# A routed-expert stage in a three-stage kernel: two buffers for the split relu output, three PSUM banks for y, unused tiles signalled ahead of the last product with w2, last y stores by SyncE

## What is computed

```python
# stage A: attention, half the heads with a plain window of 32, half with a dilated one
scores = where(mask, q @ k.T / 8, -1e9); x = softmax(scores) @ v      # -> (4, 576, 512)
# stage B: a router with memory, then one expert of 8 for each token
e = argmax(logits) if s == 0 or sigmoid(x @ w_local) < 0.5 else prev_e
h = maximum(x[b, s] @ w1[e], 0.0)        # 512 -> 1024
out[b, s] = p[e] * (h @ w2[e])           # 1024 -> 512
# stage C: a gated projection
gate = sigmoid(causal_conv(x, conv_w, 5 taps)); y = (gate * (x @ w_val)) @ w_out
```

## Time and profile before

| | us |
|---|---|
| median of 3 runs | 605.35 |
| lowest, highest | 600.86, 609.49 |
| the profiled execution | 606.63 |
| its span, first to last instruction | 604.9 |
| TensorE busy | 550.4 (91%) |
| VectorE, ScalarE, GpSimd busy | 265.5, 214.9, 246.6 |
| mean granted clock of TensorE | 0.955 of full speed |

### The profile page before, as it was taken

One profiled execution on the slowest core, in us unless ns is written; L12 is line 12 of the kernel. 1 busy time (PEld: TensorE's weight loads), 2 busy tenths in 40 slices (PEclk: granted clock), 3 DMA queues, 4 the chain that ended last, 5 costly groups with the idle time before them and its releaser, 6 DMA issues.

```text
span 604.9 us, 9972 instructions
## 1 busy us (share of the span) xinstructions
PE 550.4 (91%) x3274; PEld 466.9 (77%) x3274; DVE 265.5 (44%) x833; ACT 214.9 (36%) x478; POOL 246.6 (41%) x145
## 2 busy tenths in 40 slices
PE   7899999974789997999999999999699587999997
PEld 3789899862568886788888888878587386999986
DVE  4577777745722122021212221221112579998720
ACT  3577777741012112121212121221112454665421
POOL 1000000471177466636175577575743526522210
PEclk9799999985899999799999999999999788999999
DMA  5758489868179996978588797999761522210112
GB/s 179 183 167 223 138 267 321 278 200 264 35 225 388 308 334 241 357 291 294 177 309 287 263 356 262 351 285 350 234 222 33 170 54 65 75 62 36 53 66 91
DMA packets 62516, 128.42 MB, mean 212 GB/s; under 512 B 9408, under 2 KB 17600, under 8 KB 61952
## 3 DMA queue, kind: packets, MB, share of 16 engines
q1 hardware_dynamic: 38560, 68.43, 34.9%
q0 software_dynamic: 17136, 46.93, 24.3%
q10 hardware_dynamic: 6768, 12.36, 6.0%
HBM read 104.28 MB, written 23.41 MB: 211 GB/s over the span
## 4 chain that ended last, share of the span: by engine, by line
PE 44%; DMA 25%; POOL 14%; issue 7%; DVE 7%; SPq 2%; ACT 1%; POOLq 0%; ACTq 0%; PEldq 0%; DVEq 0%
PE bank L1159 26%; POOL w_low L566 10%; DMA w_high<-in_moe_w 8%; DMA stage<-in_moe_w 7%; PE bank L1176 6%; PE bank L1197 4%; DMA x_sorted<-gathered 3%; POOL gathered L602 2%; PE bank L1185 2%; DMA kT<-in_k 2%; DVE gate_acc L972 2%; PE bank L1220 2%; DMA gathered<-x_tokens,token_idx 1%; DMA vwin<-in_v 1%; PE bank L1372 1%
## 5 line engine op out<-in xcount | busy, mean ns | idle before, releaser
L566 POOL TENSOR_TENSOR w_low<-stage,w_high 128x2048 fp32r<-128x2048 f32 x32 | 146.5, 4587 | 98.9 <-DMA stage<-in_moe_w 56.6
L1159 PE MATMUL bank<-w_high,x_high 128*128 x184 | 75.6, 411 | 13.2 <-POOL w_low L566 10.6
L1015 ACT ACTIVATE probs<-shifted,negmax 96x128 f32<-96x128 f32 x192 | 66.4, 394 | 37.9 <-PE bank L1185 22.4
L1159 PE MATMUL bank<-w_high,h_high 128*128 x184 | 73.7, 401 | 1.3 <-DVE h_low L933 1.0
L1159 PE MATMUL bank<-w_high,x_low 128*128 x184 | 73.3, 398 | 0.0
L1159 PE MATMUL bank<-w_low,x_high 128*128 x184 | 73.2, 398 | 0.0
L1159 PE MATMUL bank<-w_high,h_low 128*128 x184 | 71.9, 391 | 0.0
L1159 PE MATMUL bank<-w_low,h_high 128*128 x184 | 71.8, 390 | 0.0
L919 DVE TENSOR_TENSOR x_low<-bank,x_high 128x512 fp32r<-128x512 f32 x25 | 17.3, 691 | 119.0 <-ACT x_high L1056 106.6
L1056 ACT CAST x_high<-bank 128x512 fp32r<-128x512 f32 x25 | 14.7, 587 | 154.0 <-PE bank L1283 154.0
L1072 ACT CAST h_high<-bank 128x1024 fp32r<-128x1024 f32 x25 | 25.4, 1017 | 115.6 <-PE bank L1311 108.7
(11 more groups left out here) (184 smaller groups left out, 1060.1 us busy)
## 6 DMA issues: line engine op xcount, KB each, us to landing
w_high<-in_moe_w POOLq DMA_DIRECT2D x16, 2048.0 KB, 15.0
stage<-in_moe_w SPq DMA_DIRECT2D x32, 1024.0 KB, 7.4
y_sorted<-y_sb ACTq DMA_DIRECT2D x25, 256.0 KB, 7.2
vwin<-in_v SPq DMA_DIRECT2D x4, 1560.0 KB, 7.2
x_sorted<-gathered SPq DMA_DIRECT2D x21, 256.0 KB, 16.9
x_in<-x_sorted ACTq DMA_DIRECT2D x21, 256.0 KB, 6.6
kT<-in_k SPq DMA_DIRECT2D x32, 152.0 KB, 4.7
out<-o_sb SPq DMA_DIRECT2D x18, 256.0 KB, 2.0
```

The source lines that it names most:

```text
L566: g.tensor_tensor(low, stage[:, c % 2, :], high.bitcast(F32), ALU.subtract).then_inc(split_done, 1)
L1015: a.activation(probs[:, j % 2, u, :], shifted[:, j % 2, u, :], ACT.Exp, bias=negmax[:, j % 2, u:u + 1], scale=-1.0).then_inc(exp_done, 1)
L1159: ins = mm(dst, l, r, start=first and i == 0, stop=last and i == 2)
```

## The change

- h_high and h_low get two buffers, by the parity of the tile. To make room `x_in` goes from two buffers to one, y_sb from three to two, and `logits` moves to the region `late`.
- y uses banks 5, 6 and 7 in turn; the first rows of stage C use banks 0 and 1.
- The x rows of a tile are loaded one step later. The first three tiles, not four, are gathered directly.
- VectorE copies y of tile s-3 in step s, behind h_low and x_low. ScalarE stores y of tile s-4, up to tile 21; tiles 22 to 24 are stored by SyncE inside its counting loop.
- When the first unused tile is met, TensorE signals for all unused tiles at once, ahead of the last `down`, and the ten small products stand behind that `down`'s waits.

```diff
-DIRECT = 4
+DIRECT = 3
-YB = 3
+YB = 2
+ACT_STORES = TOKENS // 128 + EXPERTS - 4
+LAG = 3
...
-        x_in = small("x_in", [128, 2, MODEL], F32)
+        x_in = small("x_in", [128, MODEL], F32)
-        h_high = small("h_high", [128, FF], F32R)
-        h_low = small("h_low", [128, FF], F32R)
+        h_high = small("h_high", [128, 2, FF], F32R)
+        h_low = small("h_low", [128, 2, FF], F32R)
...
-            return i % 2 + (6 if i < NQ else 0)
+            return i % 2
+        def y_bank(tile):
+            return 5 + tile % LAG
...
             for tile in range(ST):                                  # SyncE
+                if tile >= ACT_STORES:
+                    sp.wait_ge(y_copied, tile + 1)
+                    sp.dma_start(ys_dram[tile * 128:(tile + 1) * 128, :], y_sb[:, tile % YB, :]
+                                 ).then_inc(y_stored[tile % YB], 16)
+                    settle(sp)
                 sp.wait_ge(y_stored[tile % YB], 16 * (tile // YB + 1))
                 sp.sem_inc(y_count, 1)
...
             def gather_direct(tile):                                # GpSimd
-                if tile >= 2:
-                    po.wait_ge(xin_transposed, tile - 1)
+                if tile >= 1:
+                    po.wait_ge(xin_transposed, tile)
...
             gather_direct(1)
+            gather_sorted(0)
             gather_direct(2)
-            gather_sorted(0)
-            gather_direct(3)
...
             def copy_y(tile):                                       # VectorE
+                dve.wait_ge(tiles_done, tile + 2)
                 if tile >= YB:
                     dve.wait_ge(y_stored[tile % YB], 16 * (tile // YB))
...
-                if y_before:
-                    dve.wait_ge(tiles_done, s)
-                    copy_y(s - 2)
                 dve.wait_ge(hid_high, s)
...
-                if x_next:
+                if s < ST - 1:
                     low_x(s + 1)
+                if s >= LAG:
+                    copy_y(s - LAG)
...
-            def load_x(half, parity):                               # ScalarE
-                s = 2 * half + parity
-                act.wait_ge(xin_transposed, s - 1)
+            def load_x(s):
+                act.wait_ge(xin_transposed, s)
...
+            def tile_step(s):
                 act.wait_ge(hidden_transposed, s)
+                if s >= 3:
+                    act.wait_ge(tiles_done, s - 1)
+                if s >= 2:
+                    act.wait_ge(hid_split, s - 1)
+                a.copy(h_high[:, (s - 1) % 2, :].rearrange("p (g n) -> p g n", g=2), bank[:, 3:5, :]
+                       ).then_inc(hid_high, 1)
+                if DIRECT <= s + 1 < ST:
+                    load_x(s + 1)
+                if s >= LAG + 1 and s - LAG - 1 < ACT_STORES:
+                    store_y(s - LAG - 1)
...
-            def down(s):                                            # TensorE
+            def down(s, settling=False):
                 pe.wait_ge(hid_split, s + 1)
-                if s > 0:
-                    pe.wait_ge(y_copied, s)
+                if s >= LAG:
+                    pe.wait_ge(y_copied, s - LAG + 1)
                 e = expert_of(s)
                 pe.wait_ge(split_done, CHUNKS * e + CHUNKS)
+                if settling:
+                    for _ in range(10):
+                        mm(bank[:, y_bank(s), 0:128], ident[:], ident[:], start=True, stop=True)
...
                 with pe.Else():
-                    pe.sem_inc(ups_done, 1)
-                    if s + 1 < ST:
-                        pe.wait_ge(xin_split, s + 1)
-                        pe.sem_inc(xin_transposed, 1)
                     with pe.If(used > s - 1):
-                        for _ in range(10):
-                            mm(bank[:, 6, 0:128], ident[:], ident[:], start=True, stop=True)
-                        down(s - 1)
-                    with pe.Else():
-                        pe.sem_inc(tiles_done, 1)
-                    pe.wait_ge(tiles_done, s + 1)
-                    pe.wait_ge(hid_split, s)
-                    pe.sem_inc(hidden_transposed, 1)
+                        pe.wait_ge(xin_transposed, s + 1)
+                        pe.wait_ge(hidden_transposed, s)
+                        pe.sem_inc(ups_done, ST - s)
+                        if s + 1 < ST:
+                            pe.sem_inc(xin_transposed, ST - s - 1)
+                        pe.sem_inc(hidden_transposed, ST - s)
+                        down(s - 1, settling=True)
+                        pe.wait_ge(tiles_done, s + 1)
+                        pe.sem_inc(tiles_done, ST - s)
...
+            pe.wait_ge(xin_split, ST)
+            pe.wait_ge(hidden_ready, ST)
             for i in range(NQ):
                 transpose_rows(i)
             pe.wait_ge(out_weights, 2)
+            pe.wait_ge(hid_split, ST)
             pe.wait_ge(y_copied, ST)
```

More of the change, by code:

```diff
@@ L90, in build @@
         KIB = 1024
-        always = Region(base, 4 * KIB)
-        late = Region(base + 4 * KIB, 32 * KIB)
-        stage_at = base + 36 * KIB
+        late_at = base + 1792
+        always = Region(base, 1792)
+        late = Region(late_at, 32 * KIB)
+        stage_at = late_at + 32 * KIB
         high_at = stage_at + 16 * KIB
@@ L117, in build @@
         x_plain = late("x_plain", [QB, NQ, MODEL // 2], F32)
+        logits = late("logits", [QB, TT, EXPERTS + 1], F32)
         kT = hole("kT", [128, PAIRS, 2, WINDOW + SEQ], F32)
@@ L132, in build @@
         warm = rest("warm", [128, 512], BF16)
-        table = Region(base + 4 * KIB, 32 * KIB)
+        table = Region(late_at, 18 * KIB + 1536)
         fixed = Region(rest.at, rest.end - rest.at)
@@ L286, in build @@
         sorted_ready = sem("sorted_ready")
-        xin_direct = [sem(f"xin_direct{i}") for i in range(2)]
-        xin_loaded = [sem(f"xin_loaded{i}") for i in range(2)]
+        xin_direct = sem("xin_direct")
+        xin_loaded = sem("xin_loaded")
         xin_transposed = sem("xin_transposed")
@@ L616, in gather_direct @@
             def gather_direct(tile):
-                if tile >= 2:
-                    po.wait_ge(xin_transposed, tile - 1)
-                gather(x_in[:, tile % 2, :], tile).then_inc(xin_direct[tile % 2], 16)
+                if tile >= 1:
+                    po.wait_ge(xin_transposed, tile)
+                gather(x_in[:, :], tile).then_inc(xin_direct, 16)
             gather_direct(0)
             gather_direct(1)
+            gather_sorted(0)
             gather_direct(2)
-            gather_sorted(0)
-            gather_direct(3)
             load_high(1, 1, 0)
@@ L941, in _ @@
             sum_probs()
-            tile_step(1, y_before=False)
-            for s in range(2, ST + 1):
-                tile_step(s, x_next=s < ST - 1)
-            dve.wait_ge(tiles_done, ST + 1)
-            copy_y(ST - 1)
+            for s in range(1, ST + 1):
+                tile_step(s)
+            for tile in range(ST - LAG + 1, ST):
+                copy_y(tile)
             def plain_c(i):
@@ L1067, in store_y, with tile_step @@
                 act.dma_start(ys_dram[s * 128:(s + 1) * 128, :], y_sb[:, s % YB, :]).then_inc(y_stored[s % YB], 16)
[L1069 to L1070 removed]
+            def tile_step(s):
                 act.wait_ge(hidden_transposed, s)
[L1072 to L1077 removed]
+                if s >= 3:
[9 more added lines that the diff above has]
+                if s + 1 < ST:
                     high_x(s + 1)
[L1079 removed]
+                if s < ST:
                     relu(s)
@@ L1085, in _ @@
             relu(0)
-            tile_step(0, 1, x_load=False, y_before=False)
-            for s in range(2, ST + 1):
-                tile_step(s // 2, s % 2, x_load=s + 2 < ST, x_next=s + 1 < ST)
-            store_y(ST - 1)
+            for s in range(1, ST + 1):
+                tile_step(s)
             def high_c(i):
@@ L1329, in tile_step @@
                 if s + 1 < ST:
[L1330 removed]
+                    transpose_x(s + 1)
                 down(s - 1)
                 transpose_hidden(s)
[L1334 removed]
+            transpose_x(0)
             up(0)
[L1336 removed]
+            transpose_x(1)
             slot_probabilities()
```

46 lines of the change are left out of this document (18 added, 28 removed).

## The result

The changed kernel takes 630.85 us at the median of 7 runs (629.75 to 645.15), against 605.35 (600.86 to 609.49, 7 runs) for the kernel before: ratio 1.0429, 95% interval 1.0385 to 1.0473, or 23.3 to 28.6 us. The forecast was 621 with a range of 611 to 631. The direction is right; the size is 9.9 us short, and the result stands at the range's upper end (630.85 at the median, 631.3 by the ratio). The execution profiled with this result was a slow one such as several of these kernels show now and then (645.15), so the rows here are of a second profile of the same kernel, after_again (627.47 us, span 625.7); the ratios leave such executions out, and so differ from the quotient of the medians, in shorter_tail most, where the ratio rests on 4 of 12.

What follows compares the result with a forecast made beforehand. By stage, the prediction took TensorE's work with waits for split weights in the experts' tiles, then the seam, as the bound. Tiles 6.4, settling 2.4 and seam 6.9 made +15.7 on 605.35, so 621 us, range 611 to 631.

Steps and rivals of the forecast that it cites:

- What bounds the kernel now: Whole kernel, judged by stage: the change touches only the experts' tiles (about 165 to 472 us) and the seam after.
- the x_in part: Tiles' stage: loads with 5.20 us to land beside weights make TensorE wait 0.5 to 2.7 us, about 1.0 a step.
- all 9.2 are absorbed: Steps 7 to 22: the 9.2 us of waits for weights of experts 6 and 7 cover part of the load cost.
- the T0 term, +6.4: Tiles' stage: the h_high cast after the last used tile (T0) moves by 16.0 - 9.2 - 0.4 = +6.4 us.
- they are hidden: Steps 2 to 5: four late loads at 1.4 us (5.6) vanish under step 6's existing 7.0 us wait.
- 16 x 1.0: Steps 7 to 22: 16 loads cost 1.0 us each, 16.0, with about 3 in 10 quiet; ends 0.3 and 1.4 each.
- The settling products, +2.4: Before the last used down product: ten small products, now behind the h_low wait, add 2.4 us; slow clock up to 2.8 more.
- The seam, +6.9: Last used product to ScalarE's first cT copy: tile 21's store held, gathers and pads later, +6.9 us (ends +0.7, +9).
- A: Rival, tiles' stage: loads arrive in time and only the seam costs, 605.4 + 9.3 = 614.7 us; chance 0.13.
- D: Rival, tiles' stage landings: lighter DMA queues remove the weight waits, -6.9 us, 598.5, so not slower; chance 0.05.
- C: Rival, seam: early signals cost nothing, as batch 0 doesn't need tile 21's store; 614.7 us; chance 0.09.
- B: Rival, steps and seam: no load is quiet and the clock falls at the seam, +24.9 us, 630; chance 0.13.

Runs made afterwards that it cites:

- after_again: The changed kernel, unedited, run and profiled again; 633.13 us at the median, ratio 1.049 to the kernel before.
- shorter_tail: Changed kernel; x load half a step earlier, tile 21's copy and store and settling products ahead of waits, pads memset on VectorE, unused tiles' copies later; 606.89 us, ratio 0.991.
- late_load_without_weights: Kernel before, x load one step later, weight loads from the third expert on cut to 64 columns of one row block; 602.24 us, ratio 0.992.
- last_store_ahead: The changed kernel with tile 21's store ahead of ScalarE's wait for the last product; 629.19 us, no ratio formed.
- x_load_half_step_earlier: The changed kernel, one x_in buffer kept, each x load issued behind relu of the step before; 616.14 us, ratio 1.016.
- before_with_late_load: The kernel before, two x_in buffers kept, with each x load asked for one step later; 621.65 us, ratio 1.026.

## Why the prediction came out as it did

- **What bounds the kernel now: right.** The tiles' stage and the seam, and nothing else, moved.
- **The mechanism of the x_in part: right.** The late load costs because it lands beside the weights (shown by late_load_without_weights, whose issue is as late), and the waits for w_low are absorbed: 10.9 us became 0.7, as "all 9.2 are absorbed" said. The way back was seen too: with the load early again, w_low waits 10.2.
- **The step that failed is the T0 term, +6.4, and in it the first six steps: "they are hidden", of the loads ahead of step 6.** T0 moved by 10.6 in the profiles. Step 7 was to start 0.4 us sooner; steps 1 to 6 took 4.2 us more (83.2 against 79.0). That is 4.6 us off, and T0 as a whole is 4.2 off. Of the 4.6, 2.8 are dearer waits: the forecast gave steps 1 to 6 80.4 us (257.5 - 177.1), with 1.4 for each early load and 1.0 in step 6. In after_again steps 2 and 3 lost 1.8 and 4.7 us, and step 6, freed of its weight wait, lost 3.9 to its own x_in. Behind the waits of steps 3 and 6 the clock was at its lower level for a while, and so it was in step 3 of all five late-loading executions. In after_again the granted clock is 0.51 over 217.4 to 220.6 us, which loses some 1.6 us (an estimate: half of 3.2). The forecast let TensorE arrive in step 6 "without the hole and the slow clock" and priced no clock loss in the load term. The other 1.8 lie in the profile that it was worked from: its steps 1 to 6 took 80.8 us, where four executions with an early load have 79.0, so there was less waiting to hide in.
- **"16 x 1.0": right in size, by errors that cancel.** Steps 7 to 22 hold 16.4 us over 12.25 each in the mean of the five, where 16.0 was forecast, and 6.7 net of the weights' waits, where 6.8 was. But the share of loads that wait was put at 7 in 10 and is 6 of 16 in after_again (9 of 21 in all), and one wait was priced at the landing minus 5.20, 1.4 us. It costs the wait (15.3 / 9 = 1.7), the register load exposed behind it (3.7 / 9 = 0.4), and behind some of them products at the lower clock: steps 1 to 22 hold 24.0 us over 12.25 each, 0.7 of it the wait for w_low, and 23.3 / 9 is 2.6 us a wait (2.1 in steps 7 to 22). That the two cancel is luck.
- **The earlier trace rows was read as all 21 loads, and is of ten.** The view's 5.7 / 6.6 / 7.9 us are the loads of odd tiles. The other eleven count on another semaphore, two of whose 176 landings aren't in the trace, and the view leaves such a group out: asked for a single load of an even tile, it gives no landing. The records that are there make 2.8 to 7.9 us for all 21, 6.4 at the median. Of the 16 issued in steps 7 to 22 ten took 6.2 us or more, 1.6 over 5.20 in the mean, and six landed within 3.8. So "3 in 10 are quiet", a guess from one y store, was near for the kernel before (6 of 16).
- **The medians say more than the profiles.** The late load alone gave 17.0 us (11 to 20, so the term's upper end of 12.8 isn't excluded), where its profile shows 11.0. What makes up the rest stays open.
- **The settling products, +2.4: right in the kernel profiled (+2.1)**, and 3.5 in the mean of three, as the twenty rows take 3.72 us in last_store_ahead and 2.49 in after_again. The forecast named that clock loss and kept it outside the term.
- **The seam, +6.9: right.** 7.1 measured, through the chain named: h_high held by the last product, the store behind it, the first gather at T1 + 3.2 (forecast 3.0), the pads done 9.7 us later (forecast 9.7).
- **The rivals.** A (loads in time) and D (lighter queues) fall with the nine waits. C (early signals cost nothing) falls to the gather that started at T1 + 3.2, not under the product. B stood at 630, which is what was measured, but of its "no load is quiet" the trace shows the opposite, 12 of 21 in time, and the clock loss that it put at the seam lies mostly in the steps. The right number there has the wrong reason.

What stays open: why fewer of the late loads land late, though both are issued right behind h_high (over 5.20 us: 15 of 21 in the kernel before, and 9 of 22 in after_again and 7 of 21 in before_with_late_load), and how much of the 25.5 us is the chance spread of the waits, which is wider with a late load (23.1 to 29.8 us over 12.25 a step in steps 1 to 22) than with an early one (14.0 to 17.0).

## What to carry to other kernels

When a load is moved nearer to its use, price a late arrival by the whole stall of the waiting queue: the wait, what the sequencer could no longer read ahead, and the products at the lower clock behind it. Here that was some 2.6 us for 1.7 of waiting. How often it waits can't be read from the old landings: here their median fell from 6.4 to 4.2 us with the change itself, so both ends have to stay in the range. Ask how many transfers a median of landings stands on; one here stood on ten of 21. And don't call a cost hidden under a wait that was measured in one execution only. And before a signal is given early, list what is queued behind the next instruction that waits on the same engine: one parked store cost 7 us at this seam, and the edit that takes this back moves one call.

## What the hardware showed that I had not expected

- A stall of 2.0 us ahead of four transposes was enough for slow products behind it: the granted level fell from 2.4 to 1.2 GHz (0.39 to 0.63 us a product) from 217.4 to about 220.6 us in after_again. Such stretches aren't new with the change: in steps 1 to 22 the five late-loading executions spend 6.8 to 13.7 us at the lower level, and the four with an early load, whose waits are for weights, as much (10.2 in the mean of each).
- The register load that picks the expert's weights costs TensorE up to 0.8 us when its sequencer arrives at it after a wait for x_in (nine gaps, 3.7 us in all, in after_again); moved ahead of the wait, no such gap was left.
- The same 256 KB load landed in 2.5 us at best (x_load_half_step_earlier) and 9.4 at worst (before_with_late_load: 2.8 / 4.4 / 9.4). With the weights gone and the DMA share at 0.24 the median was 3.0.
- The unchanged kernel enters the tiles' stage at 177.1 us in one execution and 184.5 in another. A difference of that size between the T0 of two single profiles says nothing.
